# One kernel on Trainium2: expert weights in scaled fp16 halves, with the first matrix as the stationary operand

## The chip, the cores and the metric

The kernel runs on one core of a Trainium2 chip, as one program and one launch. The metric is the device time of an execution in microseconds (us); the result has to match the reference in float32.

## What is computed

Three parts follow one another: attention with 4 sink tokens and a window of 128, a dense MLP, and a mixture of 8 experts of which each token takes one. The change touches the third, with a piece of the second.

```python
# x: 3072 tokens x 512, out of attention (4 batches, 8 heads, 768 positions, head size 64)
h = x @ w_in; x = (h - np.tanh(h)) @ w_out           # 512 -> 2048 -> 512
logits = x @ w_gate + modality_bias[modality_id]     # 8 experts
e_idx = np.argmax(logits, axis=1); gate_w = ...      # softmax value of the chosen one
for e in range(E):
    mask = e_idx == e
    if not mask.any():
        continue
    h = np.maximum(x[mask] @ w1[e], 0.0)             # 512 -> 1024
    out[mask] = gate_w[mask, None] * (h @ w2[e])     # 1024 -> 512
```

With the inputs given, two of the eight experts get tokens, 1550 and 1522 of them.

## The kernel before

Attention and the dense MLP run in one block of 8 chunks (windows `w` = 0 to 7) of 384 tokens. A chunk has 32 slots `k`; in every second one an MLP step `f` begins: PE computes h_ps (L703), ACT takes tanh (L715), DVE the difference (L724), ACT and DVE its high and low fp16 halves (L734, L744), and PE adds g times w_out (L759). The routing of the chunk before, and attention of the next one, run beside it. SP's queue loads the eight raw pieces of the first expert's weights (`raw0` to `raw7`, 128x1024 float32, four of w1 and four of w2) in the last chunk.

Then comes the routing's end and a plan on DVE: `plan_blocks` and `plan_late` fill small tables (`meta`, `meta_late`) that tell for every block of 128 tokens which slots, which expert turn, and whether new weights are to be prepared. The block "experts" follows. Its engines take turns by semaphores; the order on each is that in which `iteration` calls the steps:

- `load_slots`, `gather` (POOL): slot numbers from DRAM, then an indirect DMA of 128 token rows into `xg`. `carry_waits` is a tiny POOL operation on `tick` that holds a wait before a DMA.
- `transpose_x`: 4 PE transposes into xt_ps (L1467), ACT copies the high part (L1472), DVE the remainder (L1475).
- `prep`: the weights of the next expert, split into a high and a low part in fp32r, ACT `w_hi` (L1429), DVE or POOL `w_lo` (L1432).
- `hidden` (L1498): 24 matmuls of 512 columns, tokens stationary, weights moving: low x high, high x low, high x high for each quarter of the depth and each half of the width.
- `hidden_transpose`: relu on ACT and DVE into `hid` (L1506, L1508), 8 transposes (L1519), and the halves `hid_hi` (L1527) and `hid_lo` (L1530).
- `output` (L1545): 24 matmuls of 512 columns, ACT scales by the gate value (L1551), POOL scatters the rows (L1556).

In an iteration `j` hidden of block `j` stands ahead of output of block `j - 1`. The weights lie in a buffer with two halves, chosen at run time: `par` is the parity of the expert turn, read from a table on each engine with `value_load` (helper `read`, L1405). A matmul on such a buffer takes its address from a register that instructions of the same engine compute. The loop is

```python
            with eng.Fori(2, NB) as j:       # L1605, NB = 31
                with eng.If(j <= last):      # L1606
                    block_step(E, eng, j)
```

`last` is 24 here (25 blocks), so that 6 passes of the loop are empty. In the tables of this document PE's queue of such instructions is PEldq, DVE's DVEq; FUSED_REGOPS and ALU_OP are register instructions, TENSOR_LOAD is the load of a table value.

Of the kernel before, what the change touches and what calls it, by code (L numbers as in the profile page):

```python
# [48 lines left out]
NB = NT + NE - 1  # L49
# [50 lines left out]
def attention_buffers(sb):  # L100
# [12 lines left out]
    words = 4 * QK + 2 * CT + 4 * KR + NB2 * DM + 2 * NB2 * HP * VW + 3 * DM + RING * KW + 6 * KW + 3 * P + 15 * P  # L113
    return (qk_raw, q_stack, kh_stack, kl_stack, v_raw, v_hi, v_lo, vs_raw, vs_hi, vs_lo, probs, normed, sinks, pt_hi, pt_lo), words


def front(nc, dram, shared, attention):

    with ExitStack() as ctx:
# [37 lines left out]
        ident = sb("ident", [P, P], F32)  # L157
# [743 lines left out]

        def gate_last(E, eng, g):
# [215 lines left out]
        def window(E, eng, w, first):  # L1118

            i = first  # L1120
            for k in range(SLOTS):
# [121 lines left out]
class Shared:  # L1243


    def __init__(self, sb, sem):
# [3 lines left out]
        self.early_int = sb("early_int", [1, 1], I32)  # L1250

# [10 lines left out]

    def over_attention(self, sb):

        self.raw = [sb(f"raw{i}", [P, FE], F32) for i in range(PIECES)]
        self.iota_t = sb("iota_t", [1, NT], F32)
# [8 lines left out]
        return PIECES * FE + NT + MB + NE + TURNS + 4 * MB + 5 * TURNS + TURNS * NT + 2 * MB * TURNS + 5 * MB  # L1275
# [15 lines left out]
    def plan(self, E, eng, counts):  # L1291
# [23 lines left out]
        step(ts(mv["active"][:], mv["blocks"][:], 0.0, None, ALU.is_gt))  # L1315
        step(eng.tensor_tensor_scan(mv["end"][:], self.one_x[:], mv["blocks"][:], 0.0, ALU.mult, ALU.add))
# [28 lines left out]
    def plan_late(self, eng):  # L1345
# [7 lines left out]
        first, now, b = vec["first"], metaf[:, 2, :], vec["b"]  # L1353
        step(ts(vec["t"][:], first[:], -1.0, 1.0, ALU.mult, ALU.add))
        step(ts(metaf[:, 2, :], first[:], 0.0, None, ALU.mult))
        step(tt(now[:, 1:MB], first[:, 0:MB - 1], first[:, 1:MB], ALU.mult))
        step(tt(b[:, 2:MB], first[:, 0:MB - 2], vec["t"][:, 1:MB - 1], ALU.mult))
        step(tt(now[:, 2:MB], now[:, 2:MB], b[:, 2:MB], ALU.add))
# [3 lines left out]
        step(tt(now[:, 1:MB], now[:, 1:MB], b[:, 0:MB - 1], ALU.mult))  # L1362
# [8 lines left out]
def experts(nc, dram, shared):  # L1371
# [5 lines left out]
    with ExitStack() as ctx:  # L1377
        sb, ps, sem = allocators(nc, ctx)
        tick, raw, q_raw = shared.tick, shared.raw, shared.raw_in
        w1_hi, w1_lo = (sb(n, [P, 2, KD, FE], F32R) for n in ("w1_hi", "w1_lo"))  # L1380
        w2_hi, w2_lo = (sb(n, [P, 2, KF, DM], F32R) for n in ("w2_hi", "w2_lo"))
# [3 lines left out]
        xg_hi, xg_lo = (sb(n, [P, DM], F32R) for n in ("xg_hi", "xg_lo"))  # L1385
        hid = sb("hid", [P, FE], F32)
        hid_hi, hid_lo = (sb(n, [P, FE], F32R) for n in ("hid_hi", "hid_lo"))
        y = sb("y", [P, DM], F32)
        ident = sb("ident2", [P, P], F32)
# [3 lines left out]
        ht_ps = [ps(f"ht_ps{i}", [P, 512], F32) for i in range(2)]  # L1393
        y_ps = ps("y_ps", [P, DM], F32)

        names = ("ident slot_in gathered xt_done xt_hi xt_lo "
                 "hid_mm relu_act relu_dve ht_done ht_hi ht_lo y_mm y_out scattered slot_y_in "
                 "ht_half carried_1 carried_2 carried_3").split()
        q = {n: sem("e_" + n) for n in names}
        q_hi, q_lo = ([sem(f"e_{x}{i}") for i in range(PIECES)] for x in ("hi", "lo"))  # L1400
# [5 lines left out]


        def load_turn(eng, s):
            e = read(eng, 3, s, NE - 1)
            for i in range(PIECES):  # L1410
                eng.wait_ge(q_lo[i], s)
                load_piece(eng, dram, shared, e, i)

        def piece(x_w1, x_w2, i, par):
            if i < KD:
                return x_w1[:, par, i, :] if isinstance(par, int) else x_w1[:, bass.ds(par, 1), i, :].rearrange("p a n -> p (a n)")
# [156 lines left out]
        def program(E, eng):  # L1573
# [13 lines left out]
            if E == "pe":  # L1587
                eng.wait_ge(q["ident"], 2)
# [108 lines left out]
```

## Time and profile before

| what | value |
|---|---|
| median of 3 runs | 1177.43 us (1176.83 to 1181.7) |
| profiled execution, its own time | 1180.4 us |
| its span | 1178.8 us |
| mean granted TensorE clock | 0.964 |
| PE busy | 1052.0 us, 89% of the span |
| PEld (weight loads) busy | 714.6 us, 61% |
| DVE busy | 690.8 us, 59% |
| ACT busy | 600.0 us, 51% |
| POOL busy | 414.6 us, 35% |

The span is that of one execution under the profiler, from the first to the last instruction. Busy times of an engine say how much it did, not whether anyone waited for it; that is told by the chain of waits, which follows the work that ended last back from the end. The whole-kernel table mixes stages: the experts take the last 350 us of it.

### The profile page before, as it was taken

The numbers are of one execution on the slowest core, as the hardware profiler recorded it, in microseconds if no ns is written. First come the engines' busy times: TensorE is split into PE (matmuls) and PEld (weight loads), VectorE is DVE, ScalarE is ACT, GpSimd is POOL, SyncE is SP. The second block draws the span as 40 slices with busy tenths as digits, with TensorE's granted clock in tenths as the row PEclk, the third lists the DMA queues.
The fourth block names the chain that finished last, engine by engine and source line by source line (L and its number), as shares of the span: only waits on it lengthen the run. The fifth ranks groups of instructions, "written<-read, shape, count | busy, mean of one in ns | idle before, by whom it ended". The sixth has DMA issues, their size and how long they took to land. (4 is left out here: it accounts for less than half of the span.)

```text
span 1178.8 us, 22058 instructions
## 1 busy us (share of the span) xinstructions
PE 1052.0 (89%) x6236; PEld 714.6 (61%) x6237; DVE 690.8 (59%) x2204; ACT 600.0 (51%) x1404; POOL 414.6 (35%) x469
## 2 busy tenths in 40 slices
PE   1667888999999999999999999995389999999996
PEld 0534554665665665665665666553277888888885
DVE  6787977678878778877777766334543222122221
ACT  2675866666686676676775765332332122122211
POOL 3796785123254223253322410002514222222221
PEclk9968999999999999999999999998689999999999
DMA  9731112312311421311321200400041111111111
GB/s 290 243 99 33 33 32 64 111 35 36 88 33 32 102 77 33 81 43 33 65 59 33 60 1 1 170 1 27 18 171 45 45 44 37 37 45 36 45 45 35
DMA packets 24245, 74.14 MB, mean 63 GB/s; under 512 B 10016, under 2 KB 10016, under 8 KB 22624
## 3 DMA queue, kind: packets, MB, share of 16 engines
q1 hardware_dynamic: 14768, 59.66, 18.9%
q0 software_dynamic: 5792, 13.43, 3.6%
q8 instruction: 40, 0.66, 0.3%
q10 hardware_dynamic: 3600, 0.03, 0.2%
q14 instruction: 45, 0.37, 0.1%
HBM read 60.04 MB, written 13.33 MB: 62 GB/s over the span
## 5 line engine op out<-in xcount | busy, mean ns | idle before, releaser
L759 PE MATMUL acc<-w_out_all,g_hi 128*128 128x512 f16 x768 | 228.3, 379 | 0.0
L703 PE MATMUL h_ps<-xt_hi,w_in_all 128*128 128x384 f16 x1024 | 211.0, 329 | 13.2 <-DVE g_raw L724 13.2
L759 PE MATMUL acc<-w_out_all,g_lo 128*128 128x512 f16 x384 | 145.4, 379 | 3.2 <-DVE g_lo L744 1.7
L703 PEld LDWEIGHTS h_ps<-xt_hi,w_in_all 128*128 128x128 f16 x1024 | 98.0, 98 | 73.1 <-issue 10.6
L591 ACT ACTIVATE pt_hi<-pt_ps 128x256 f16<-128x256 f32 (+2 forms) x224 | 83.5, 379 | 109.4 <-PE pt_ps L608 105.3
L97 POOL TENSOR_TENSOR tick<-tick 1x1 f32<-1x1 f32 x87 | 21.7, 249 | 317.1 <-ACT y L1551 114.4
L715 ACT ACTIVATE g_raw<-h_ps,batch_scale 128x384 f32<-128x384 f32 x128 | 74.2, 580 | 88.7 <-PE h_ps L703 87.4
L759 PEld LDWEIGHTS acc<-w_out_all,g_hi 128*128 128x128 f16 x768 | 75.0, 98 | 69.2
L744 DVE SCALAR_TENSOR_TENSOR g_lo<-g_raw,batch_scale,g_hi 128x384 f16<-128x384 f32 x128 | 95.1, 743 | 33.1 <-ACT g_hi L734 30.7
L595 DVE TENSOR_TENSOR pt_lo<-pt_ps,pt_hi 128x256 f16<-128x256 f32 (+2 forms) x224 | 94.3, 423 | 29.0 <-ACT pt_hi L591 27.2
L429 POOL TENSOR_TENSOR q_stack<-qk_raw,q_stack 64x768 f16<-64x768 f32 x31 | 50.8, 1637 | 165.6 <-ACT q_stack L425 165.6
L1530 DVE TENSOR_TENSOR hid_lo<-ht_ps,hid_hi 128x512 fp32r<-128x512 f32 x50 | 32.3, 686 | 127.6 <-ACT hid_hi L1527 127.6
L724 DVE SCALAR_TENSOR_TENSOR g_raw<-h_ps,batch_scale,g_raw 128x384 f32<-128x384 f32 x128 | 78.4, 613 | 48.7 <-ACT g_raw L715 47.7
L703 PE MATMUL h_ps<-xt_lo,w_in_all 128*128 128x384 f16 x512 | 106.1, 331 | 0.0
L572 ACT ACTIVATE normed<-probs,row_sum 128x260 f32<-128x260 f32 (+1 forms) x192 | 92.9, 484 | 20.5 <-DVE row_sum L567 20.4
L734 ACT ACTIVATE g_hi<-g_raw,batch_scale 128x384 f16<-128x384 f32 x128 | 78.0, 609 | 39.5 <-DVE g_raw L724 39.0
L554 ACT ACTIVATE probs<-probs,neg_max 128x260 f32<-128x260 f32 (+1 forms) x192 | 92.7, 483 | 5.8 <-DVE neg_max L549 5.7
L429 POOL TENSOR_TENSOR kl_stack<-qk_raw,kh_stack 128x1048 f16<-128x1048 f32 (+1 forms) x31 | 60.1, 1939 | 99.2 <-ACT kh_stack L425 98.9
L608 PE MATMUL pt_ps<-ident,normed 128*128 128x128 f32 x352 | 73.7, 285 | 22.3 <-ACT normed L572 22.3
L549 DVE CUSTOM_DVE_ANT_0 probs<-s_ps,mask 128x260 f32<-128x260 f32 (+1 forms) x180 | 73.1, 406 | 24.4 <-issue 23.2
L1545 PE MATMUL y_ps<-w_hi,hid_lo 128*128 x200 | 81.2, 406 | 2.6 <-DVE hid_lo L1530 2.6
L1551 ACT ACTIVATE y<-y_ps,slot_y 128x512 f32<-128x512 f32 x25 | 17.2, 687 | 124.5 <-PE y_ps L1545 124.5
(248 smaller groups left out, 2233.4 us busy)
## 6 DMA issues: line engine op xcount, KB each, us to landing
qk_raw<-in_qk SPq DMA_DIRECT2D x64, 454.0 KB, 6.0
raw<-in_w SPq DMA_DIRECT2D x16, 512.0 KB, 6.5
v_raw<-in_v SPq DMA_DIRECT2D x4, 1536.0 KB, 9.9
x_tokens<-x SPq DMA_DIRECT2D x24, 256.0 KB, 5.4
w_in_all<-in_w_in SPq DMA_DIRECT2D x4, 1024.0 KB, 13.2
w_out_all<-in_w_out SPq DMA_DIRECT2D x4, 1024.0 KB, 12.2
slot_g<-slots POOLq DMA_DIRECT2D x27, 1.0 KB, 2.0
xg<-x_tokens,slot_g POOLq DMA_INDIRECT x27, 3.4
```

What stands on the lines that cost most here:

```text
L429: eng.tensor_tensor(lo, raw[half], hi[half], ALU.subtract).then_inc(q["conv_lo"], 1)
L554: eng.activation(probs[:, r, cols], probs[:, r, cols], ACT.Exp, bias=neg_max[:, r:r + 1], scale=-1.0, accum_out=row_sum[:, r:r + 1]).then_ ...
L572: eng.activation(normed[:, u % 6, cols], probs[:, r, cols], ACT.Copy, scale=row_sum[:, r:r + 1])\
L591: eng.activation(pt_hi[:, at, :], out, ACT.Copy).then_inc(q["pt_hi_done"], 1)
L595: eng.tensor_tensor(pt_lo[:, at, :], out, pt_hi[:, at, :], ALU.subtract).then_inc(q["pt_lo_done"], 1)
L703: mm = eng.matmul(h_ps, w16[0][:, f, x * DM + k * P:x * DM + (k + 1) * P], r[:, par, k, :], start=(i == 0), stop=(i == 3 * KD - 1))
L715: eng.activation(g_raw[:, f % 2, :], h_ps, ACT.Tanh, scale=batch_scale[:, b, 0:1]).then_inc(q["tanh_done"], 1)
L724: eng.scalar_tensor_tensor(g, h_ps, batch_scale[:, b, 0:1], g, ALU.mult, ALU.subtract).then_inc(q["g_done"], 1)
L734: eng.activation(g_hi[f % 2][:], g, ACT.Copy, scale=batch_scale[:, b, 1:2]).then_inc(q["g_hi_done"], 1)
L744: eng.scalar_tensor_tensor(g_lo[f % 2][:], g, batch_scale[:, b, 1:2], g_hi[f % 2][:], ALU.mult, ALU.subtract)\
L759: mm = eng.matmul(acc[t][:, :], l[f % 2][:, t * P:(t + 1) * P], w16[1][:, f, x * DM:(x + 1) * DM], start=(f == 0 and i == 0), stop=(f == N ...
L1545: mm = eng.matmul(y_ps[:, :], l[:, f * P:(f + 1) * P], rhs, start=(f == 0 and i == 0), stop=(f == KF - 1 and i == 2))
```

## The change

Weights and activations of the experts are scaled by powers of two and kept as fp16 high and low halves. For this the kernel looks over each expert's weights (`look_over`: ACT sums squares of w1's pieces, DVE takes the largest magnitude of w2's), combines them across partitions (`sum_rows`, `spread` with two small matmuls) and makes scales (`set_scales`, eight small DVE operations). `split` makes the halves, ACT high and DVE low. Each gathered block gets a scale per token (`scale_x`), undone in the factor of the output (`output_scale`).

`hidden` now has w1 as the stationary operand and the tokens as the moving one, so its result is already transposed: 96 matmuls of 128 columns in place of 24 of 512; `hidden_transpose` is gone. `output` stands in the same iteration as its `hidden`. The first expert's weights are looked over and split in the last chunk of the MLP (`prepare_expert`, slots 9 to 21); the second expert's in `look_ahead`, `scale_ahead` and `split_ahead` over three iterations, each behind a table read and a branch. `plan_late` runs before the first iteration, and all engines wait for it. An expert with tokens gets at least two blocks, and `NB` becomes 38.

```diff
-NB = NT + NE - 1
+NB = NT + 2 * NE - 2
...
+        def prepare_expert(E, eng, k):
+
+            if k in (9, 11):
+                for i in (k - 9, k - 8):
+                    shared.look_over(E, eng, 0, i)
+            if k == 11:
+                shared.sum_rows(E, eng, 0)
+            if k == 13:
+                shared.spread(E, eng, 0, pt_bank[0])
+                shared.set_scales(E, eng, 0, pt_bank[0])
+            if k in (15, 17, 19, 21):
+                shared.split(E, eng, 0, (k - 15, k - 14))
...
+                if w == NC - 1:
+                    prepare_expert(E, eng, k)
...
+    def look_over(self, E, eng, s, i):
+
+        if E == "act":
+            eng.wait_ge(self.raw_in[i], 16 * (s + 1))
+            need(eng, self.rows_set, 2 * s)
+            eng.activation(self.junk[:, i, :], self.raw[i][:], ACT.Square, accum_out=self.sums[:, i:i + 1])\
+               .then_inc(self.squared, 1)
+        if E == "dve":
+            eng.wait_ge(self.raw_in[KD + i], 16 * (s + 1))
+            eng.tensor_reduce(self.tops[:, i:i + 1], self.raw[KD + i][:], AX.X, ALU.max,
+                              apply_absolute_value=True).then_inc(self.maxed, 1)
...
+    def spread(self, E, eng, s, bank):
+
+        if E == "pe":
+            eng.wait_ge(self.rows_set, 2 * (s + 1))
+            need(eng, self.scaled, s)
+            for i in range(2):
+                mm = eng.matmul(bank[:, P * i:P * (i + 1)], self.rows[:, i:i + 1].to_broadcast([P, P]), self.ident[:],
+                                start=True, stop=True)
+            mm.then_inc(self.spread_done, 1)
+
+    def set_scales(self, E, eng, s, bank):
+
+        if E != "dve":
+            return
+        eng.wait_ge(self.spread_done, s + 1)
...
+        step(eng.tensor_reduce(self.both[:], bank[:, 0:2 * P].rearrange("p (i n) -> p i n", i=2), AX.X, ALU.max))
+        step(ts(exps[:], self.both[:].bitcast(I32), 255 * EXP1, None, ALU.bitwise_and))
+        step(ts(exps[:, 0:1], exps[:, 0:1], float(147 * EXP1), 0.5, ALU.add, ALU.mult))
...
+        step(ts(self.w_scale[:].bitcast(I32), exps[:], -1.0, float((254 + TOP16) * EXP1), ALU.mult, ALU.add))
...
+    def split(self, E, eng, s, pieces):
+
+        for i in pieces:
+            scale = self.w_scale[:, 0:1] if i < KD else self.w_scale[:, 1:2]
+            hi, lo = (self.piece(x, i, s % 2) for x in (self.hi, self.lo))
+            if E == "act":
+                eng.wait_ge(self.scaled, s + 1)
+                eng.activation(hi, self.raw[i][:], ACT.Copy, scale=scale).then_inc(self.w_hi[i], 1)
+            if E == "dve":
+                eng.wait_ge(self.scaled, s + 1)
+                eng.wait_ge(self.w_hi[i], s + 1)
+                eng.scalar_tensor_tensor(lo, self.raw[i][:], scale, hi, ALU.mult, ALU.subtract).then_inc(self.w_lo[i], 1)
...
+        def scale_x(E, eng, j):
+
+            if E == "dve":
+                step = chain(eng, q["x_step"], 4 * j)
+                ts = eng.tensor_scalar
+                eng.wait_ge(q["gathered"], 16 * (j + 1))
+                need(eng, q["x_scaled"], j)
+                if not (isinstance(j, int) and j < 2):
+                    eng.wait_ge(q["y_set"], j - 1)
+                step(eng.tensor_reduce(x_top[:], xg[:], AX.X, ALU.max, apply_absolute_value=True))
+                step(ts(x_exp[:], x_top[:].bitcast(I32), 255 * EXP1, None, ALU.bitwise_and))
+                step(ts(x_exp[:], x_exp[:], float(2 * EXP1), float(253 * EXP1), ALU.max, ALU.min))
+                step(ts(x_scale[:].bitcast(I32), x_exp[:], -1.0, float(255 * EXP1), ALU.mult, ALU.add))
+                ts(column(x_undo, j % 2).bitcast(I32), x_exp[:], float(-EXP1), None, ALU.add).then_inc(q["x_set"], 1)
+            if E == "act":
+                eng.wait_ge(q["x_set"], j + 1)
+                eng.activation(xg[:], xg[:], ACT.Copy, scale=x_scale[:]).then_inc(q["x_scaled"], 1)
...
+        def hidden(E, eng, j, s):
+
+            for c in range(2):
+                if E == "pe":
+                    par = s % 2
+                    if c == 0:
+                        eng.wait_ge(q["xt_lo"], j + 1)
+                    if not (isinstance(j, int) and j == 0):
+                        eng.wait_ge(q["hid_lo"], 2 * j - 1 + c)
+                    for f in range(4 * c, 4 * c + 4):
+                        i = 0
+                        for x, w in ((xg_lo, shared.hi), (xg_hi, shared.lo), (xg_hi, shared.hi)):
+                            for k in range(KD):
+                                if c == 0 and f == 0 and i < KD:
+                                    eng.wait_ge(shared.w_lo[k], s + 1)
+                                mm = eng.matmul(hid_ps[c][:, (f - 4 * c) * P:(f - 4 * c + 1) * P],
+                                                shared.piece(w, k, par)[:, f * P:(f + 1) * P], x[:, k * P:(k + 1) * P],
+                                                start=(i == 0), stop=(i == 3 * KD - 1))
+                                i += 1
+                    mm.then_inc(q["hid_mm"], 1)
+                half = slice(c * 512, (c + 1) * 512)
+                if E == "act":
+                    eng.wait_ge(q["hid_mm"], 2 * j + c + 1)
+                    need(eng, q["y_mm"], j)
+                    eng.activation(hid_hi[:, half], hid_ps[c][:, :], ACT.Relu).then_inc(q["hid_hi"], 1)
+                if E == "dve":
+                    eng.wait_ge(q["hid_hi"], 2 * j + c + 1)
+                    eng.scalar_tensor_tensor(hid_lo[:, half], hid_ps[c][:, :], 0.0, hid_hi[:, half], ALU.max, ALU.subtract)\
+                       .then_inc(q["hid_lo"], 1)
...
-                    for i, (l, r) in enumerate(((hid_lo, w2_hi), (hid_hi, w2_lo), (hid_hi, w2_hi))):
-                        rhs = r[:, par, f, :] if isinstance(par, int) else r[:, bass.ds(par, 1), f, :].rearrange("p a n -> p (a n)")
+                        eng.wait_ge(shared.w_lo[KD + f // 2], s + 1)
+                    for i, (l, w) in enumerate(((hid_lo, shared.hi), (hid_hi, shared.lo), (hid_hi, shared.hi))):
+                        rhs = shared.piece(w, KD + f // 2, par)[:, (f % 2) * DM:(f % 2 + 1) * DM]
...
-        def iteration(E, eng, j, turn, turn_before):
-
-            load_slots(E, eng, j + 2)
-            prep_ahead(E, eng, j, range(KD))
-            hidden(E, eng, j, turn)
-            transpose_x(E, eng, j + 1)
-            prep_ahead(E, eng, j, range(KD, PIECES))
-            gather(E, eng, j + 2)
-            if turn_before is not None:
-                load_slots_again(E, eng, j - 1)
-                output(E, eng, j - 1, turn_before)
-            hidden_transpose(E, eng, j)
+        def iteration(E, eng, j, ago_1, ago_2):
+
+            turn = 0 if isinstance(j, int) and j == 0 else read(eng, 1, j, NE) if E in ("pe", "dve") else None
+            if E == "pe":
+                hidden(E, eng, j, turn)
+                scale_ahead(E, eng, ago_1)
+                transpose_x(E, eng, j + 1)
+                output(E, eng, j, turn)
+            if E == "act":
+                hidden(E, eng, j, turn)
+                transpose_x(E, eng, j + 1)
+                load_slots_again(E, eng, j)
+                split_ahead(E, eng, j, ago_2, range(KD, PIECES))
+                look_ahead(E, eng, j)
+                split_ahead(E, eng, j, ago_1, range(2))
+                output(E, eng, j, turn)
+                scale_x(E, eng, j + 2)
+                split_ahead(E, eng, j, ago_1, range(2, KD))
+            if E == "dve":
+                hidden(E, eng, j, turn)
+                transpose_x(E, eng, j + 1)
+                output_scale(E, eng, j, turn)
+                split_ahead(E, eng, j, ago_2, range(KD, PIECES))
+                look_ahead(E, eng, j)
+                scale_ahead(E, eng, ago_1)
+                scale_x(E, eng, j + 2)
+                split_ahead(E, eng, j, ago_1, range(KD))
...
+            if E == "dve":
+                shared.plan_late(eng)
...
             transpose_x(E, eng, 0)
             eng.wait_ge(shared.planned, 1)
             last = read(eng, 1, MB - 1, NB - 1, lo=NT - 1)
             load_slots(E, eng, 1)
             gather(E, eng, 1)
-            prep(E, eng, 0, 0, range(KD, PIECES))
-            if E == "dve":
-                shared.plan_late(eng)
-            iteration(E, eng, 0, 0, None)
-            if E in ("act", "dve", "pool"):
-                eng.wait_ge(shared.planned_late, 1)
-            block_step(E, eng, 1)
+            scale_x(E, eng, 1)
+            eng.wait_ge(shared.planned_late, 1)
+            iteration(E, eng, 0, None, None)
+            iteration(E, eng, 1, 0, None)
             with eng.Fori(2, NB) as j:
                 with eng.If(j <= last):
-                    block_step(E, eng, j)
-            load_slots_again(E, eng, last)
-            output(E, eng, last, read(eng, 1, last, NE) if E == "pe" else 0)
+                    iteration(E, eng, j, j - 1, j - 2)
             if E == "pool":
```

PE, in the loop body, within `hidden`: one k-step of before (ISA and REGISTER_ALU are register instructions; `ew_hi`, `ew_lo` are the halves of the weights).

```order
L1498 ISA
L1498 MATMUL hid_ps<-w_hi,xg_lo 128x512
L1498 ISA
L1498 MATMUL hid_ps<-w_hi,xg_lo 128x512
L1498 REGISTER_ALU
L1498 MATMUL hid_ps<-w_lo,xg_hi 128x512
L1498 REGISTER_ALU
L1498 MATMUL hid_ps<-w_lo,xg_hi 128x512
L1498 MATMUL hid_ps<-w_hi,xg_hi 128x512 x2
L1464 ISA
L1467 MATMUL xt_ps<-ident,xg 128x128 x4
```

And of the change, one of its eight groups `f`.

```order
L1602 ISA
L1602 MATMUL hid_ps<-xg_lo,ew_hi 128x128
L1602 REGISTER_ALU
L1602 MATMUL hid_ps<-xg_hi,ew_lo 128x128
L1602 REGISTER_ALU
L1602 MATMUL hid_ps<-xg_hi,ew_lo 128x128
L1602 REGISTER_ALU
L1602 MATMUL hid_ps<-xg_hi,ew_lo 128x128
L1602 REGISTER_ALU
L1602 MATMUL hid_ps<-xg_hi,ew_lo 128x128
L1602 MATMUL hid_ps<-xg_hi,ew_hi 128x128 x4
L1602 ISA
```

A step of before has 2 ISA and 2 REGISTER_ALU for 6 matmuls of 512 columns, four steps in all; the change has 4 ISA and 4 REGISTER_ALU for 12 matmuls of 128 columns, eight groups in all.

DVE, in the loop body of the change, behind xg_lo: `output_scale`, and the first of the reads of `meta_late` with its branch.

```order
L1627 ISA
L1629 ISA
L1629 TENSOR_TENSOR y_scale<-slot_y,x_undo 128x1
L1632 ISA
L1632 TENSOR_TENSOR y_scale<-y_scale,ew_undo 128x1
L1499 ISA
L1499 TENSOR_LOAD meta_late
L1499 ISA x2
L1529 COMPARE_AND_BRANCH
```

And `scale_x` in the same body.

```order
L1558 ISA
L1562 TENSOR_REDUCE x_top<-xg 128x1
L90 ISA
L1563 TENSOR_SCALAR x_exp<-x_top 128x1
L90 REGISTER_ALU
L1564 TENSOR_SCALAR x_exp<-x_exp 128x1
L90 REGISTER_ALU
L1565 TENSOR_SCALAR x_scale<-x_exp 128x1
L90 REGISTER_ALU
L1566 ISA
L1566 TENSOR_SCALAR x_undo<-x_exp 128x1
```

Neither stood on DVE before, which had two table reads in an iteration there, and now has five.

## Rows read from the trace of the kernel before

**Rows 1.** Chain of waits over the experts: start us, us, what.

```profile
837.57 3.41 DMA xg<-x_tokens,slot_g
...
846.00 6.02 DVE w_lo L1432 x2
...
858.82 8.55 PE hid_ps L1498 x24
867.80 5.61 PE y_ps L1545 x24
...
906.38 5.61 PE y_ps L1545 x24
...
924.51 0.88 PE ht_ps L1519 x8
925.39 5.61 PE hid_ps L1498 x24
930.99 0.44 PE xt_ps L1467 x4
```

**Rows 2.** Busy time by stretch: a steady period, and part of the last chunk.

```profile
core 0: us, PE busy (x) PEld busy (x) DVE busy (x) ACT busy (x) POOL busy (x), PEclk, DMA share, GB/s
950.42:962.95 12.53, 12.53 (x61) 10.23 (x61) 2.67 (x4) 2.76 (x6) 3.15 (x6) 1.00 0.14 42
...
780.00:808.00 28.00, 27.18 (x149) 14.24 (x147) 11.22 (x35) 7.70 (x15) 3.10 (x4) 1.00 0.01 1
```

**Rows 3.** PE's queue, line 1498: duration ns min/median/max, first and last start us.

```profile
L1498 PEldq FUSED_REGOPS  x8: 46/46/94, 962.2 to 963.9; - x8
L1498 PEldq ALU_OP  x8: 32/32/32, 962.5 to 964.1; - x8
```

**Rows 4.** PE's queue, line 1545, the last output; columns as in rows 3.

```profile
L1545 PEldq ALU_OP  x8: 32/32/32, 1165.9 to 1167.8; - x8
```

**Rows 5.** Timeline of PE: start us, us, engine line op out<-in xcount.

```profile
52.06 1.08 PE L279 MATMUL acc<-w_out_all 128*128 128x128 bf16 x16
52.98 0.22 PE L539 MATMUL s_ps<-kl_stack,q_stack 128*128 128x132 f16 x1
```

**Rows 6.** Timeline of a step of the last chunk, PE and ACT.

```profile
748.58 0.38 PE L759 MATMUL acc<-w_out_all,g_lo 128*128 128x512 f16 x1
...
748.78 0.58 ACT L715 ACTIVATE g_raw<-h_ps,batch_scale 128x384 f32<-128x384 f32 x1 [1.94 <-PE h_ps L703]
...
749.23 0.38 PE L759 MATMUL acc<-w_out_all,g_lo 128*128 128x512 f16 x1
...
752.67 0.58 ACT L715 ACTIVATE g_raw<-h_ps,batch_scale 128x384 f32<-128x384 f32 x1 [2.01 <-PE h_ps L703]
```

**Rows 7.** PE's queue, lines 1605 and 1405, one turn; columns as in rows 3.

```profile
L1605 PEldq ALU_OP  x1: 32/32/32, 972.3 to 972.3; - x1
...
L1405 PEldq TENSOR_LOAD <-meta x2: 298/299/300, 973.0 to 973.8; - x2
```

**Rows 8.** Groups by form on DVE: xcount, busy us, mean ns, idle before.

```profile
L1530 DVE TENSOR_TENSOR hid_lo<-ht_ps,hid_hi 128x512 fp32r<-128x512 f32 x50 | 32.3, 686 | 127.6 <-ACT hid_hi L1527 127.6
...
L452 DVE TENSOR_REDUCE v_top<-v_raw 128x1 f32<-128x512 f32 x24 | 16.3, 678 | 1.0 <-DMA v_raw<-in_v 0.8
...
L397 DVE TENSOR_SCALAR qk_scale<-qk_scale 128x1 int32<-128x1 int32 x32 | 4.9, 153 | 1.1
...
L432 DVE SCALAR_TENSOR_TENSOR kl_stack<-qk_raw,qk_scale,kh_stack 128x792 f16<-128x792 f32 x1 | 1.0, 1030 | 0.0
```

**Rows 9.** DVE's queue, line 1405, one read; columns as in rows 3.

```profile
L1405 DVEq TENSOR_LOAD <-meta_late x1: 312/312/312, 964.5 to 964.5; - x1
```

**Rows 10.** Timeline of POOL before the first gather.

```profile
833.46 3.95 POOL L97 TENSOR_TENSOR tick<-tick 1x1 f32<-1x1 f32 x1 [0.79 <-DMA slot_g<-slots]
```

**Rows 11.** Timeline of PE, the last matmul.

```profile
1171.37 0.39 PE L1545 MATMUL y_ps<-w_hi,hid_hi 128*128 x1
```

**Rows 12.** DVE's queue, line 1605, empty passes of the loop; columns as in rows 3.

```profile
L1605 DVEq ALU_OP  x6: 40/40/40, 1164.9 to 1168.5; - x6
```

More of the change, by code:

```diff
@@ L1261, in __init__ @@
         self.blocks_step = sem("plan_blocks_step")
+        self.squared = sem("squared")
+        self.maxed = sem("maxed")
+        self.rows_set = sem("rows_set")
+        self.spread_done = sem("spread_done")
+        self.scale_step = sem("scale_step")
+        self.scaled = sem("scaled")
+        self.w_hi = [sem(f"ew_hi{i}") for i in range(PIECES)]
+        self.w_lo = [sem(f"ew_lo{i}") for i in range(PIECES)]
     def over_attention(self, sb):
         self.raw = [sb(f"raw{i}", [P, FE], F32) for i in range(PIECES)]
+        self.hi, self.lo = (sb(n, [P, 2, PIECES, FE], F16) for n in ("ew_hi", "ew_lo"))
+        self.junk = sb("junk", [P, KD, FE], BF16)
+        self.sums = sb("sums", [P, KD], F32)
+        self.tops = sb("tops", [P, PIECES - KD], F32)
+        self.rows = sb("rows", [P, 2], F32)
+        self.both = sb("both", [P, 2], F32)
+        self.exps = sb("exps", [P, 2], I32)
+        self.w_scale = sb("ew_scale", [P, 2], F32)
+        self.undo = sb("ew_undo", [P, TURNS], F32)
         self.iota_t = sb("iota_t", [1, NT], F32)
@@ L1350, in plan_late @@
         turns = mv["turn_end"][:, TURNS - 1:TURNS]
[L1353 to L1358, printed above, removed]
+        b = vec["b"]
         step(ts(b[:], metaf[:, 1, :], 1.0, None, ALU.add))
@@ L1361, in plan_late @@
         step(tt(b[:], b[:], vec["t"][:], ALU.mult))
-        step(tt(now[:, 1:MB], now[:, 1:MB], b[:, 0:MB - 1], ALU.mult))
+        step(tt(metaf[:, 2, :], vec["first"][:], b[:], ALU.mult))
         step(tt(grid["a"][:], mv["turn_end"][:].unsqueeze(1).to_broadcast([1, MB, TURNS]), self.iota_j[:].unsqueeze(2).to_broadcast([1, MB, TURNS]), ALU.is_le))
@@ L1378, in experts @@
         sb, ps, sem = allocators(nc, ctx)
-        tick, raw, q_raw = shared.tick, shared.raw, shared.raw_in
-        w1_hi, w1_lo = (sb(n, [P, 2, KD, FE], F32R) for n in ("w1_hi", "w1_lo"))
-        w2_hi, w2_lo = (sb(n, [P, 2, KF, DM], F32R) for n in ("w2_hi", "w2_lo"))
+        tick, ident = shared.tick, shared.ident
         slot_g = sb("slot_g", [P, 2], I32)
@@ L1510, in hidden_transpose, with output_scale @@
[L1510 to L1531 removed]
+        def output_scale(E, eng, j, s):
+            if E == "dve":
+                eng.wait_ge(q["slot_y_in"], 16 * (j + 1))
+                need(eng, q["y_out"], j)
+                eng.tensor_tensor(y_scale[:], slot_y[:, 1:2].bitcast(F32), column(x_undo, j % 2), ALU.mult)\
+                   .then_inc(q["y_step"], 1)
+                eng.wait_ge(q["y_step"], j + 1)
+                eng.tensor_tensor(y_scale[:], y_scale[:], column(shared.undo, s), ALU.mult).then_inc(q["y_set"], 1)
@@ L1549, in output @@
                 eng.wait_ge(q["y_mm"], j + 1)
-                eng.wait_ge(q["slot_y_in"], 16 * (j + 1))
-                eng.activation(y[:], y_ps[:, :], ACT.Copy, scale=slot_y[:, 1:2].bitcast(F32)).then_inc(q["y_out"], 1)
+                eng.wait_ge(q["y_set"], j + 1)
+                eng.activation(y[:], y_ps[:, :], ACT.Copy, scale=y_scale[:]).then_inc(q["y_out"], 1)
             if E == "pool":
@@ L1591, in program @@
             gather(E, eng, 0)
-            prep(E, eng, 0, 0, range(KD))
+            if E == "dve":
+                shared.plan_late(eng)
+            scale_x(E, eng, 0)
             transpose_x(E, eng, 0)
```

166 lines of the change are left out of this document (63 added, 103 removed).

## The prediction

> **What bounds the kernel now.** I read the page, then the chain of waits over the experts, then single queues. The chain shows a part to 829.8 us that the change hardly touches, a start in which conversions are in the way, and a steady state where one TensorE group follows another: hid_ps 5.61, y_ps 5.61, ht_ps 0.88, xt_ps 0.44 us, so 12.52 us per block of 128 tokens [rows 1]. In one such period PE is busy throughout, at a granted clock of 1.00, with DVE at 2.67 us, ACT at 2.76 and POOL at 3.15 [rows 2]. The array bounds the blocks; whatever takes columns off it pays until another limit is reached. The next one can be seen: the sequencer that feeds PE. For the 24 hidden matmuls it carries out 16 register instructions (8 FUSED_REGOPS, 8 ALU_OP), from 962.2 to 964.1, some 2.02 us with the last matmuls [rows 3]. The last output, where nothing holds it, takes it 2.4 us for as many (the ALU_OPs start from 1165.9 to 1167.8 [rows 4]). Now it does this ahead of an array that needs 5.61 us.
>
> **The array after the change.** Hidden: 96 matmuls of 128 columns for 24 of 512, the same 12,288 columns, each with a weight load of its own. Static 128-column bf16 matmuls with their own loads run 16 from 52.06 to 52.98, 57 ns apart [rows 5]: 96 x 0.057 = 5.5 us for 5.61. Output: an fp16 matmul of 512 columns takes 0.216 us, three from 748.58 to 749.23 [rows 6], for 0.234: 24 x 0.216 = 5.2, a gain of 0.4. The ht_ps transposes go, 0.88. The array needs 5.5 + 5.2 + 0.44 = 11.1 us per block for 12.52.
> The Trainium skill, page "TensorE: Matmul & The Clock Gate", section "Back-to-back issue gap", gives about 81 ns per matmul for a stream of load and matmul pairs at 128 columns. Row 5 says 57; the page's figure is weighed among the rivals.
>
> **The sequencer after the change.** In the new order each group of 12 hidden matmuls carries 4 ISA and 4 REGISTER_ALU, so 64 for 96 matmuls where there were 16 for 24: everything is fourfold. So I need not split the cost between register instructions and matmuls: 4 x 2.02 = 8.1 us [rows 3], and 4 x 2.4 = 9.6 if the output's pace holds [rows 4]. The rest of its period: loop turn 0.6 (from 972.3 to the next read, whose load starts at 973.0 [rows 7]), a table read, 0.8, since two TENSOR_LOADs start 0.8 apart [rows 7], with 0.3 of address work behind it; in the middle the new read and branch of scale_ahead, which PE does nowhere yet, taken at a read and 0.2 for the branch, 1.0; waits and xt_ps 0.2; output 2.4. Sum 0.6 + 0.8 + 0.3 + 8.1 + 1.0 + 0.2 + 2.4 = 13.4 us. The array's backlog cannot help: it has its 11.1 us done while the sequencer takes 13.4. **Period 13.4 us.** From below 12.6, with 4 x 1.9 for hidden (first to last start [rows 3]) and 0.8 for the read and branch, 0.1 off the rest; from above 15.0, by 9.6 and the waits.
>
> **Other engines in the period.** DVE: two hid_lo and xg_lo 3 x 0.69 [rows 8], five reads with their branches 4.6 (its TENSOR_LOAD takes 312 ns [rows 9], PE's 299 in a read of 0.8; with a branch I take 0.92), scale_x 0.68 for the 512-wide reduce [rows 8] and four small operations at 0.2 (153 ns and a gap [rows 8]), y_scale 0.4, loop 0.7: 9.3 us, under 13.4. ACT has as many reads and five operations of DVE's length or less, and is no longer. The new chain of gather (3.41 us to land [rows 1]), scale_x 1.5, multiply 0.6 starts at xt_ps of one block and has until the next: 6 us of slack. Output can no longer lie a block behind hidden; what covers its hid_lo (ACT 0.6, DVE 0.69, 1.5 us with waits) is the read, xt_ps and the first half of output, 2.4 us of sequencer time. Cost nothing, up to 0.3 if that cover is thin.
>
> **The last chunk.** DVE gets two looks or two splits over 128x1024 (1.2 and 1.3 us, estimates by the reduce of 512 columns at 0.68 and the two-operand form of 792 at 1.03 [rows 8]) in slots 9, 11, 15, 17, 19 and 21. One MLP step of two slots is 3.89 us (tanh to tanh [rows 6]), and from 780 to 808 DVE is busy 11.22 of 28 [rows 2], 2.3 us free per step; but it lies in two gaps of under 2 us, before g_raw and before g_lo, for which PE waits. 2.4 to 2.6 us of work overfills it by 0.3 to 0.6 us, five or six times: **+2.5 us**, between 0.5 and 5. ACT's squares and copies at 1.0 are less. The raw loads are there before slot 9.
>
> **The start of the experts.** Now the first gather waits for a tick of 3.95 us beside DVE's w_lo [rows 10], then 3.41 for the landing; DVE has w_lo until 852.0, then plan_late; y_ps(0) ends at 873.4 [rows 1]. After: no tick held (-3.7), scale_x +2.1, xt and converts 2.4: hidden(0) from about 842.3, with static addresses; it and output(0) take 5.5 + 5.2 us and about 1 for a clock that has fallen (hid_ps(1) took 8.55 for 5.61 [rows 1]): y(0) ends near 854.1. Plan_late now runs during the gather, shorter by five operations, but every engine waits for it.
> Then the second expert's weights: SP can load only after plan_late, DVE gets 4 looks, sums and scales, and 8 splits: 4 x 1.2 + 2.1 + 8 x 1.3 = 17.3 us over blocks 1 to 3. With 9.3 of its own per block that is 3 x 9.3 + 17.3 = 45.2, part of it under block 0; I take 44.2 for these three, where 3 x 13.4 = 40.2: y(3) ends at 898.3, with the last chunk's 2.5 at **900.8**. Before it ends at 912.0 [rows 1], after a stall for POOL's w_lo and a late gather. Gain 11.2 us, between 7 and 15.
>
> **The 21 blocks from there.** Before: 912.0 to the last y_ps's end at 1171.8 [rows 1, 11], 259.8 us (20 periods and a last output by itself). After: 21 x 13.4 = 281.4. **+21.6**; 264.6 to 315 by the bounds, +5 to +55.
>
> **The tail.** Before: 7.0 us from the last matmul to the end at 1178.8 [rows 11], through ACT's y and POOL's scatter. NB is now 38, so 13 empty passes for 6. On DVE an empty pass is 0.71 us (from 1164.9 to 1168.5 for six starts [rows 12]), formerly under the last output. Now output is inside the loop: DVE has four reads and scale_x after hid_lo, done about 3 us behind the last matmul, then 13 x 0.71 = 9.2, then 1 to leave: 13.4. **+6.4**, between 3 and 8. PE's 13 x 0.73 from its sequencer's lead gives less.
>
> **Sum.** -11.2 + 21.6 + 6.4 = +16.8 us (2.5 of the last chunk is in the first term). On the profiled execution, span 1178.8 and 1180.4 in all, that is 1195.6 of span. The median of the runs shown is 1177.43, 3 us below it; the difference carries over: 1177.4 + 16.8 = **1194 us**.
>
> **Rivals.**
> *The array stays the bound (faster).* The sequencer's 2.02 us were measured while it could run, but it may be paced there by a full queue of matmuls rather than by register work. For: alone, a FUSED_REGOPS is 46 ns and an ALU_OP 32 [rows 3], and 64 of them at 40 ns are 2.6 us, less than the array's 5.5. Against: the 16 starts in 1.9 us are an even 0.12 apart, in a sequencer that is then ahead of the array, and the last output, where its queue was empty, is no faster [rows 3, 4]. It decides below 0.09 us per register instruction (8.1 would be 5.8, the array's pace). Then the period is 11.1 to 12.0 (hid_lo's latency shows): 21 x 11.6 = 244, -16, with stalls of blocks 1 to 3 unchanged -11.2, tail +6.4: 1156, 1150 to 1166. Chance 0.14.
> *A cheaper sequencer.* Period 12.5 to 12.95, around the low bound: 1175 to 1185 (each 0.1 us of it is 2.1). Chance 0.14.
> *Pairs are paced by the weight load.* If each fp16 pair with other operands than row 5's took half as long again, hidden would be 96 x 0.08 = 7.7 us and the array 13.3: 1192, hardly another time by another mechanism, told by even spacing of the matmuls with no gaps at register instructions. Chance 0.07, in the forecast's range. The page named above gives this: 96 x 81 ns = 7.8 us.
> *Dearer issue.* Pace of row 4 in hidden, or code fetched anew each turn, since a PE turn has twice the instructions: period 14 to 15, 1207 to 1228. Chance 0.13. Or the granted clock falls from 1.00 with the gaps.
> *The two-block rule for an expert* changes nothing here: the inputs give 1550 and 1522 tokens to two experts, 13 and 12 blocks, so no padding block comes. The change does what it says.
>
> **How the numbers follow.** Forecast (period 13.0 to 13.9) 0.52, with the load-paced rival 0.59; cheaper 0.14; dearer 0.13; array-bound 0.14. The range leaves out the array-bound case and the top of the dearer one: 1168 to 1212. 0.5% is about what a measurement of this kernel can tell from none. Faster by over 0.5% (below 1171.5): 0.14; slower (above 1183.3): the forecast, load-paced, dearer, and 0.02 of the cheaper: 0.74; within: 0.12.
>
> **What would show it.** Right: in a steady period hid_ps matmuls in bursts with gaps, their group 7.5 to 8.5 us long, PE's register instructions of the hidden line 64 per block at 0.12 us, PE idle put down to issue, y_ps 5.2 us, y_ps starts 13.4 apart; ACT and DVE waiting for PE; y(3) ending near 901; 13 DVE passes closing the span. Wrong: hid_ps in 5.5 us; a period under 12.5; DVE named as releaser of hid_ps in the steady state; chunk 7 longer than 3 us more or unchanged; a stall at blocks 1 to 3 over 10 us.

## The result: 1195.8 us, and the profile after

The changed kernel takes 1195.81 us in the median of 4 runs (1191.55 to 1199.68), the kernel before 1177.26 (1176.83 to 1181.7). The ratio is 1.0148, with a 95% interval of 1.0105 to 1.0191: slower by 1.5%. The forecast was 1194 us, 1168 to 1212, with a chance of 0.74 for slower. The profiled execution took 1196.78 us with a span of 1195.0, for which the prediction had 1195.6.

| | before | after | forecast |
|---|---|---|---|
| experts begin | 829.8 | 832.1 | +2.5 |
| y_ps(0) ends | 873.4 | 863.3 | 856.6 |
| y_ps(3) ends | 912.0 | 904.9 | 900.8 |
| period of a block | 12.52 | 13.21 | 13.4 |
| last y_ps ends | 1171.8 | 1182.4 | 1182.2 |
| from there to the end | 7.0 | 12.6 | 13.4 |

On the profile's page of the changed kernel PE is busy for as long as before, to 0.3%, in a span that is 16 us longer.

```profile
span 1195.0 us, 27235 instructions
...
PE 1048.7 (88%) x7844; PEld 684.4 (57%) x7845; DVE 731.0 (61%) x2392; ACT 620.8 (52%) x1422; POOL 401.1 (34%) x463
```

The chain of waits in the steady state (start us, us, what). It answers to [rows 1]: ht_ps is gone and y_ps is shorter, but hid_ps takes 6.58 us for 5.61, and 0.81 us of issue stand behind it.

```profile
984.19 6.58 PE hid_ps L1602 x96
990.77 0.81 issue
991.58 0.63 PE xt_ps L1577 x4
992.21 5.18 PE y_ps L1646 x24
```

The same period by windows (PE, PEld, DVE, ACT, POOL busy, PEclk, DMA share, GB/s). PE now has gaps, at a clock of 1.00; no other engine is busy for more than 3.7 us (register instructions and branches are not counted as busy), for 3.15 us before [rows 2].

```profile
core 0: us, PE busy (x) PEld busy (x) DVE busy (x) ACT busy (x) POOL busy (x), PEclk, DMA share, GB/s
992.21:1005.44 13.23, 12.39 (x125) 8.99 (x124) 3.70 (x10) 3.20 (x5) 3.15 (x6) 1.00 0.13 40
```

One `hidden` in PE's timeline. A row is four matmuls; the rows of `xg_lo,ew_hi` open one of the eight groups of 12 each. From 985.37 to 986.04 and 986.71 a group takes 0.67 us, 55.8 ns a matmul. From then on the groups stand 0.94, 0.98 and 0.99 us apart: what the sequencer had put in the queue is used up, and the array goes at the sequencer's pace. Within such a group the matmuls with register instructions ahead of them take 0.38 and 0.39 us for four (988.63 to 989.01 to 989.40). The last four, which have none of their own, take 0.22, the pace of the array.

```profile
985.37 0.39 PE L1602 MATMUL hid_ps<-xg_lo,ew_hi 128*128 128x128 f16 x4
...
986.04 0.39 PE L1602 MATMUL hid_ps<-xg_lo,ew_hi 128*128 128x128 f16 x4
...
986.71 0.41 PE L1602 MATMUL hid_ps<-xg_lo,ew_hi 128*128 128x128 f16 x4
...
987.65 0.45 PE L1602 MATMUL hid_ps<-xg_lo,ew_hi 128*128 128x128 f16 x4
...
988.63 0.45 PE L1602 MATMUL hid_ps<-xg_lo,ew_hi 128*128 128x128 f16 x4
989.01 0.55 PE L1602 MATMUL hid_ps<-xg_hi,ew_lo 128*128 128x128 f16 x4
989.40 0.38 PE L1602 MATMUL hid_ps<-xg_hi,ew_hi 128*128 128x128 f16 x4
989.62 0.45 PE L1602 MATMUL hid_ps<-xg_lo,ew_hi 128*128 128x128 f16 x4
```

PE's queue in that stretch (duration ns min/median/max, first and last start us), which answers to [rows 3]: 22 register instructions start within 2.6 us, 0.12 us for each on average, with their matmuls in between.

```profile
L1602 PEldq ALU_OP  x12: 32/32/32, 987.9 to 990.2; - x12
...
L1602 PEldq FUSED_REGOPS  x10: 46/46/46, 987.6 to 989.7; - x10
```

The start, in the chain of waits. Block 1's gather takes 6.99 us to land, for the 3.72 of block 0's and the 3.41 of [rows 1], and y_ps(0) runs 7.04 us for 5.18. The granted clock was 0.51 from 845 to 850 and 0.50 from 857 to 860, in the first parts of hid_ps(0) and y_ps(0), and 1.00 in the steady state.

```profile
845.68 6.99 DMA xg<-x_tokens,slot_g
852.70 0.70 DVE x_top L1562
...
856.23 7.04 PE y_ps L1646 x24
863.27 6.65 PE hid_ps L1602 x96
...
899.73 5.18 PE y_ps L1646 x24
```

The end: the last matmul, and DVE's loop instruction in its 13 empty passes and the exit, 0.69 us apart. It answers to [rows 11, 12].

```profile
1181.98 0.38 PE L1646 MATMUL y_ps<-ew_hi,hid_hi 128*128 x1
```

```profile
L1717 DVEq ALU_OP  x14: 40/40/40, 1185.6 to 1194.6; - x14
```

### The profile page after: what moved, and what is told of

Read it like the earlier page. It is cut to its first block and busy times, and to the rows that moved or that the text cites. A ratio compares the mean times of both kernels' runs of the same rounds, so it can differ in the third digit from the quotient of the medians.

```text
span 1195.0 us, 27235 instructions
## 1 busy us (share of the span) xinstructions
PE 1048.7 (88%) x7844; PEld 684.4 (57%) x7845; DVE 731.0 (61%) x2392; ACT 620.8 (52%) x1422; POOL 401.1 (34%) x463
## 5 line engine op out<-in xcount | busy, mean ns | idle before, releaser
L97 POOL TENSOR_TENSOR tick<-tick 1x1 f32<-1x1 f32 x87 | 17.2, 198 | 349.9 <-DVE payload L878 113.5
L1602 PE MATMUL hid_ps<-xg_hi,ew_lo 128*128 128x128 f16 x800 | 95.8, 219 | 0.0
L1614 DVE SCALAR_TENSOR_TENSOR hid_lo<-hid_ps,hid_hi 128x512 f16<-128x512 f32 x50 | 34.3, 691 | 91.8 <-ACT hid_hi L1611 91.8
L1602 PE MATMUL hid_ps<-xg_lo,ew_hi 128*128 128x128 f16 x800 | 85.1, 222 | 1.5 <-DVE xg_lo L1585 1.5
```

Of the source, the lines that this page charges most:

```text
L1602: mm = eng.matmul(hid_ps[c][:, (f - 4 * c) * P:(f - 4 * c + 1) * P], shared.piece(w, k, par)[:, f * P:(f + 1) * P], x[:, k * P:(k + 1) * P ...
```

## Experiments

"Fixed" below is an address known when the program is built. Times of single executions stand beside 1180.53 us for the kernel before on the same chip (1180.33 in the second set, 1178.95 in the third). Single executions of the changed kernel lie up to 8 us apart (1191.55 to 1199.68), so that a few us in the time of one say little; periods, which repeat over some 20 blocks within 0.1 us, say more.

**All of hidden at fixed addresses**

```diff
-                    par = s % 2
+                    par = 0
```

> The changed kernel, but hidden always takes its weights from the first half of the buffer, at addresses known when the program is built (so the second expert's tokens are multiplied by the first expert's w1). Its 64 register instructions per block go; output keeps its 16. My theory, that PE's sequencer sets the period of 13.2 us: it has some 8 us per block left or less, the array 11.1, so y_ps starts come 11.1 to 11.8 us apart and the time falls by 30 to 48 us, to about 1155. Rival, that pairs of weight load and 128-column matmul are slow in themselves: period 13.0 to 13.3, no change in time.

1155.22 us; y_ps starts are 11.25 to 11.29 us apart. Its chain of waits:

```profile
994.33 5.36 PE hid_ps L1602 x96
999.69 0.13 issue
999.82 0.63 PE xt_ps L1577 x4
1000.45 5.18 PE y_ps L1646 x24
```

Only the addresses have changed, and with them the 64 register instructions per block are gone: hid_ps takes 5.36 us, 96 matmuls at 55.8 ns, with 0.13 of issue behind them. The matmuls themselves are not slow. The rival of slow pairs falls. So does any by which another engine sets the period: ACT, DVE and POOL do the same work as in the changed kernel, in 11.27 us.

**Two of eight groups at fixed addresses**

```diff
-                                                shared.piece(w, k, par)[:, f * P:(f + 1) * P], x[:, k * P:(k + 1) * P],
+                                                shared.piece(w, k, 0 if f in (3, 7) else par)[:, f * P:(f + 1) * P], x[:, k * P:(k + 1) * P],
```

> As the last, but only two of hidden's eight groups have fixed addresses: 48 register instructions for 64. Sequencer theory: a fixed group costs 0.3 to 0.7 us of it for 0.98 now, so the period falls by 0.6 to 1.3 us, to 11.9 to 12.6, and the time by 13 to 29 us. Rival of slow pairs: no change.

1158.85 us, period 11.49 to 11.60, below the 11.9 to 12.6 that I expected. In the chain of waits hid_ps and the issue behind it are still over the level of the array:

```profile
994.33 5.50 PE hid_ps L1602 x96
999.83 0.19 issue
1000.02 0.63 PE xt_ps L1577 x4
1000.64 5.18 PE y_ps L1646 x24
```

As some issue time is left, the sequencer still bounds this kernel or nearly so. Sixteen register instructions less save 13.21 - 11.55 = 1.66 us, at least 0.104 us each. A fixed group of 12 then costs the sequencer at most 0.98 - 0.83 = 0.15 us, 0.83 being eight register instructions at 0.104. The matmuls that I carried along in "everything is fourfold" are a small part of it. "Register instruction" stands here for the instruction together with the matmul that takes its address; what each of the two costs alone isn't shown.

**Four of eight groups at fixed addresses**

```diff
-                                                shared.piece(w, k, par)[:, f * P:(f + 1) * P], x[:, k * P:(k + 1) * P],
+                                                shared.piece(w, k, 0 if f % 2 else par)[:, f * P:(f + 1) * P], x[:, k * P:(k + 1) * P],
```

> Four of the eight groups with fixed addresses, 32 register instructions. Sequencer theory: twice the step of the run with two groups, until the array's 11.1 us end it: period 11.1 to 12.0. Rival of slow pairs: no change. A fall that is not in proportion before the array's level would speak for a queue effect and against a fixed price per register instruction.

1156.47 us, period 11.25 to 11.31 (in these three runs the fixed groups take the first expert's w1 for both experts, so that its part for the second expert is left out). The second 16 instructions bring 0.25 us, since the array's level is reached: 5.36 + 5.18 + 0.63 and a gap of 0.1. Period against register instructions of hidden is 13.21 (64), 11.55 (48), 11.30 (32), 11.27 (0): a fall and then a floor, as with two resources of which the slower one counts. Only two of the points lie above the floor, so that a fixed price per register instruction isn't shown.

**Hidden written twice, behind a branch on the parity (everything computed)**

`hidden_of` is PE's part of `hidden` with the half of the buffer as a constant.

```diff
...
+                    with eng.If(s % 2 < 1):
+                        hidden_of(eng, j, s, 0)
+                    with eng.If(s % 2 > 0):
+                        hidden_of(eng, j, s, 1)
```

> The changed kernel with hidden written twice, for each half of the buffer with fixed addresses, and a branch on the parity that takes one of them; everything is computed. Sequencer theory: like the run with the fixed half, plus some 0.3 us for two branches that the backlog covers: period 11.1 to 11.9, time 1150 to 1168, ratio to the kernel before 0.975 to 0.99. Rival of slow pairs: ratio as for the change, 1.015. If longer code makes instruction fetch late, the gain shrinks and PE idles behind the branch by over 0.5 us per block.

1156.88 us (4 runs), ratio to the kernel before 0.9795 (0.977 to 0.9819): faster than both kernels. The period is 11.53 to 11.58 us in blocks of the first expert and 11.25 to 11.30 in those of the second. For the first expert the second body is jumped over behind hidden, where the queue is running empty:

```profile
996.25 5.36 PE hid_ps L1600 x96
1001.61 0.34 issue
1001.95 0.65 PE xt_ps L1577 x4
```

0.34 us of issue here, and 0.08 for the second expert, for which the jump lies ahead of hidden, where the backlog of y_ps covers it.

**The loop's end read at run time**

```diff
-            with eng.Fori(2, NB) as j:
-                with eng.If(j <= last):
-                    iteration(E, eng, j, j - 1, j - 2)
+            with eng.Fori(2, last + 1) as j:
+                iteration(E, eng, j, j - 1, j - 2)
```

> The changed kernel with the loop's end at last + 1, read at run time, in place of NB = 38 with a test in every pass: no empty passes. If the 13 empty passes on DVE make the tail, the time from the last matmul to the end falls from 12.6 us to 4 to 5, and the time by 8 to 11 us in all, with up to 0.2 us less per pass. If the scatter and its drain make the tail: 7 us or more stay.

1192.12 us, 1190.4 of span: 4.6 us less, for the 8 to 11 that I expected. Period 13.13 to 13.18, 0.05 less. From the last matmul to the end it is 7.0 us, as in the kernel before and not the 4 to 5 of my expectation. So the empty passes cost 5.6 us, and behind them stood, unseen, the scatter with its drain. Tail and periods make 6.7 us; 2.2 of them went at the start, where y_ps(3) began at 901.95 for 899.73 in this one execution.

**The kernel before with 13 empty passes**

```diff
-NB = NT + NE - 1
+NB = NT + 2 * NE - 2
```

> The kernel before with NB = 38: 13 empty passes instead of 6. There they run under the last output, so that seven more at 0.7 us end at about 1173.5 on DVE, ahead of the drain at 1176: 0 to +0.5 us behind the last matmul. The rival, that an empty pass costs its 0.7 us anywhere: +5 us.

1186.78 us, a span of 1185.2 for 1178.8: +6.4 us where I expected 0 to 0.5. I had looked at DVE. PE's timeline shows that the last output, which stands behind the loop, has to wait for PE's own empty passes, the last at 1169.2, with a table read behind them. It begins 14.31 us behind the output before it, for 9.10 in the kernel before:

```profile
1161.58 1.04 PE L1519 MATMUL ht_ps<-ident,hid 128*128 128x128 f32 x8
1170.45 0.79 PE L1545 MATMUL y_ps<-w_hi,hid_lo 128*128 x1 [7.83 <-issue]
1171.04 0.63 PE L1545 MATMUL y_ps<-w_lo,hid_hi 128*128 x1
```

PE is idle for 7.83 us, and its first matmuls after that are 0.43 us apart instead of 0.234, at a granted clock of 0.50 (1170.5 to 1174.4).

**Block 1's scale behind block 0's hidden**

```diff
-            scale_x(E, eng, 1)
             eng.wait_ge(shared.planned_late, 1)
...
                 hidden(E, eng, j, turn)
+                if isinstance(j, int) and j == 0:
+                    scale_x(E, eng, 1)
                 transpose_x(E, eng, j + 1)
```

> The changed kernel with the scale of block 1's tokens taken after block 0's hid_hi and hid_lo instead of before, so that block 0 does not wait for the 6.99 us landing of block 1's gather. y_ps(0) starts 2.5 to 4 us earlier, at 852 to 853.7 for 856.23. If DVE's work for the second expert sets blocks 1 to 3, under 2 us of it are left at the end of y_ps(3) (904.9 now); if not, all of it.

1199.19 us. In this run all started 1.8 us later; from the first matmul of hid_ps(0) to that of y_ps(0) it took 11.4 to 11.6 us, as before (844.65 to 856.23 there). I had expected it 2.5 to 4 us sooner. The chain of waits names who is late:

```profile
854.59 0.69 DVE x_top L1562
...
856.05 0.73 ACT xg L1569
...
856.83 1.12 PE xt_ps L1577 x4
857.95 6.08 PE y_ps L1646 x24
```

On PE the transposes of block 1 stand ahead of output(0), so that the late gather holds output in any order of DVE and ACT.

**The first expert prepared at the start of the experts**

```diff
-                if w == NC - 1:
-                    prepare_expert(E, eng, k)
...
+            for i in range(KD):
+                shared.look_over(E, eng, 0, i)
+            shared.sum_rows(E, eng, 0)
+            shared.spread(E, eng, 0, stat_ps)
+            shared.set_scales(E, eng, 0, stat_ps)
+            shared.split(E, eng, 0, range(PIECES))
```

> The changed kernel without the first expert's preparation in the last chunk: looks, scales and splits come at the start of the experts, before the first tokens are scaled. The experts begin 2.0 to 2.5 us earlier (832.1 now, about 829.8 then); DVE has 17 us of weight work ahead of scale_x(0), so hidden(0) starts at 856 to 860 for 844.7: the time rises by 8 to 13 us. If the chunk's DVE work had been free, the first part would show no difference.

1208.18 us, 11.3 more in the span. The experts begin at 829.6, hid_ps(0) at 859.53. As expected: in these two executions this part of the change costs 2.5 us where it stands and saves 14.9 at the start of hidden.

**All of PE's block written twice, with the loop's end at run time**

`side` is hidden, scale_ahead, the transposes and output on PE, with the half of the buffer as a constant.

```diff
...
+                with eng.If(turn % 2 < 1):
+                    side(eng, j, turn, 0, ago_1)
+                with eng.If(turn % 2 > 0):
+                    side(eng, j, turn, 1, ago_1)
...
+            with eng.Fori(2, last + 1) as j:
```

> The changed kernel with all of PE's work of a block written twice, once for each half of the weight buffer with fixed addresses, behind a branch on the parity, and the loop's end at last + 1 instead of empty passes. Sequencer theory: the array alone sets the period, 11.2 to 11.35 us for both experts (11.54 and 11.26 with hidden alone written twice, where the skipped body's branch fell into the gap before xt_ps); against that run 12 x 0.27 = 3 us less, and 5.6 us less at the tail, as the run with the loop's end showed: 1146 to 1150, ratio to the kernel before 0.970 to 0.977. If the branch costs as much elsewhere, the first expert's period stays at 11.5.

1144.9 us (5 runs, 1142.8 to 1146.08), ratio to the kernel before 0.9714 (0.9692 to 0.9736), about 1 us below what I expected. The period is 11.25 to 11.31 for both experts, the gap before xt_ps 0.12:

```profile
987.52 5.36 PE hid_ps L1600 x96
992.88 0.12 issue
993.00 0.63 PE xt_ps L1577 x4
993.63 5.18 PE y_ps L1649 x24
```

This is the best version: 51 us below the changed kernel, 34 below the one before. The jump over the other body, now behind y_ps, does not show in the period of either expert.

**The same, with the second expert's loads behind block 1's gather**

```diff
                 eng.wait_ge(shared.planned_late, 1)
+                eng.wait_ge(q["gathered"], 32)
```

> As two_sides, but SP loads the second expert's weights only when block 1's tokens have landed. The landing of block 1's gather then takes 3.4 to 4 us for 6.99, and y_ps(0) starts 2.5 to 3.5 us earlier after hid_ps(0) starts (8.1 to 9 us for 11.6). Whether it is kept: if DVE's work for the second expert sets blocks 1 to 3, y_ps(3) ends no earlier, and the later loads may cost up to 2 us; else 2 to 3 us less in all.

1149.2 us (4 runs), ratio to the kernel before 0.9746 (0.972 to 0.9772): 4 us worse than the version before it. The landing is short, 4.2 us from its issue at 843.6, and y_ps(0) starts at 852.57, 8.3 us behind hid_ps(0), as expected. But the loads now begin at 849.5. The small slot_y transfer beside them takes 7.21 us, DVE, which needs it for y_scale, comes to its four looks and to block 2's scale later, and y_ps(1) starts only at 870.0, for 864.9 in the version before:

```profile
853.49 7.21 DMA slot_y<-slots
...
870.01 7.02 PE y_ps L1649 x24
```

What block 0 gained, blocks 1 to 3 paid back and more; here it is right to load early.

**The kernel before with the loop's end at run time**

```diff
-            with eng.Fori(2, NB) as j:
-                with eng.If(j <= last):
-                    block_step(E, eng, j)
+            with eng.Fori(2, last + 1) as j:
+                block_step(E, eng, j)
```

> The kernel before with the loop's end at last + 1 in place of NB = 31 with a test in every pass. Its last output stands behind the loop on PE, so that the empty passes held it (with 13 of them PE sat idle 7.83 us ahead of it, and its first matmuls ran at half the clock): now y_ps(24) starts 1 to 2 us sooner, ratio 0.998 to 1.0. If the six passes cost nothing today, no difference. Either way it stays 20 us or more above the changed kernel with fixed addresses.

1178.03 us (10 runs), ratio 0.9983 (0.9964 to 1.0002): no difference that can be told from none. y_ps(24) starts 7.91 us behind y_ps(23), for 9.10 (1156.79 to 1165.89) in the kernel before, 1.2 us sooner:

```profile
1164.29 0.50 PE L1545 MATMUL y_ps<-w_hi,hid_lo 128*128 x1 [1.44 <-DVE hid_lo L1530]
```

So the loop's end is worth about 1 us to the kernel before by its trace, within what the times can tell, and the best version stays 33 us below it. In the changed layout the same edit takes away the 5.6 us that the empty passes had added there.

## Why the prediction was right, step by step

**The sequencer bounds the period: right, and shown.** The forecast was 13.4 us, measured 13.21. The runs with 48, 32 and no register instructions in hidden tell it from slow pairs: on the same matmuls the period goes to 11.27. One sign that I had named did not come: hid_ps was to be 7.5 to 8.5 us long, and it is 6.58, with 0.81 of issue behind it. The sequencer begins hidden while the array still works off y_ps, so that the first four of its eight groups run at the array's pace. The array's 11.1 us were 5.36 + 5.18 + 0.63 = 11.17. "Everything is fourfold" gave 8.1 us for hidden; eight groups at 0.98 are 7.8. The 0.2 us of error are that, with the rest of the sequencer's turn at 5.4 for 5.3. Scaling by four held for a reason that I had not separated: register instructions at 0.10 us or more carry nearly all of it, fixed matmuls almost nothing. It would have failed for a change that multiplies one and not the other.

**The rival by which the array stays the bound** named the right level (11.1 to 12.0) for the state without that work. Its argument was wrong: 46 and 32 ns are what the records show, and the price in the stream is 0.10 to 0.12 us.

**Slow pairs.** They take 55.8 ns per load and matmul of 128 columns in fp16, near the 57 that [rows 5] had for bf16. The Trainium skill, page "TensorE: Matmul & The Clock Gate", section "Back-to-back issue gap", has about 81 ns for such a stream; the runs disagree, and the measurement decides.

**The last chunk: right by luck for the start of the experts, too low for the chunk.** The experts begin 2.3 us later, for 2.5. But from the tanh at 741.04 to that at 803.16 it is 62.1 us before, and from 739.66 to 805.88 it is 66.2 after, so 4.1 us for my 2.5. By the prediction's own list, "chunk 7 longer than 3 us more" was a sign of being wrong. The looks and splits were sized right on DVE (1.21 and 1.28 us each, for 1.2 and 1.3); what they push out of a step was taken too low. The changed kernel's chunk had begun 1.4 us earlier in its run, and this hid most of it. The chunk is 62.1 us in all four profiles without this part and 66.2 in all nine with it, while its beginning moves by up to 4 us among the nine; why stays open. Single steps took up to 5.8 us for 3.9, as here with 5.1:

```profile
768.54 0.58 ACT L714 ACTIVATE g_raw<-h_ps,batch_scale 128x384 f32<-128x384 f32 x1 [0.18 <-PE h_ps L702]
...
773.68 0.58 ACT L714 ACTIVATE g_raw<-h_ps,batch_scale 128x384 f32<-128x384 f32 x1 [3.00 <-PE h_ps L702]
```

The run without that part, whose chunk takes 62.1 us and whose experts begin at 829.6, shows that it is the cause. That it is DVE's share and not ACT's is argued from the gaps, not shown.

**The start: one term missing, one too low.** hid_ps(0) began at 844.65, where the forecast with the chunk's 2.5 gives 844.8 (842.3; its terms as written add up to 841.8). y_ps(0) ended 6.7 us later than forecast. I had not priced block 1's gather beside the second expert's loads, which plan_late now releases earlier (6.99 us; some 3 us of wait; 4.2 us in the run that holds these loads back, which shows that they are the cause). The half clock I had priced at 1 us in all; it came in both hid_ps(0) and y_ps(0), 8.0 and 7.04 us for 5.5 and 5.2. Blocks 1 to 3 won part of it back: they took 41.6 us for 44.2. DVE's four looks and eight splits for the second expert took 4.6 and 9.8 us, for 4.8 and 10.4. Net y_ps(3) was 4.1 us later, and the gain 7.1 us for 11.2, at the low bound.

**The tail: right by its number, incomplete in its causes.** +5.6 for +6.4. The empty passes of DVE set it (its terms, 3 + 9.2 + 1, add up to 13.2 us and not to the 13.4 written there; measured 12.6). In the kernel before I took the empty passes for hidden under the last output. They were not: PE's own passes delayed the start of that output against the run without any, by 1.2 us with six and by 6.4 with 13. The six are part of the measured time before, and so the forecast did not suffer.

**The sum.** -7.1 + 17.7 + 5.6 = +16.2 us of span, for -11.2 + 21.6 + 6.4 = +16.8. The terms were off by +4.1, -3.9 and -0.8 us, and the first two cancelled: that the number came this close is luck, and it is better than the working. The direction is not luck: the largest term, 17.7 us, is 21 times the longer period, and the runs show what makes it longer.

## What to carry to other kernels

Count the instructions that an engine's sequencer must carry out beside those for the array, and price the turn as a whole from a stretch in which the queue was free. Matmuls on a smaller tile with run-time addresses multiply them, here from 16 to 64 in hidden. Where the run-time value has two cases, two bodies with fixed addresses behind a branch on it take that work away, and the jump belongs where the array still has a backlog. Empty passes of a loop count on every engine that has work behind the loop, not only on the last to leave.

## What the runs showed of the hardware that was not expected

- Register instructions on PE, each with the matmul that takes its address, cost the stream 0.10 to 0.12 us though their records show 32 to 46 ns; a pair of load and matmul at fixed addresses costs the sequencer at most 0.0125 us (0.15 us for 12), worked out from the periods 13.21 and 11.55.
- An idle stretch of 7.83 us on PE was followed by matmuls of 512 columns 0.43 us apart for ten of them, at a granted clock of 0.50, then 0.23 at 1.00: the wait cost another 2 us.
- A gather of 128 rows took 6.99 us beside eight loads of 512 KB, 3.4 to 4.2 without them; a transfer of 1 KB took 7.21 beside them, 1.7 at the last block of the changed kernel.
- A branch that jumps over 96 matmuls cost 0.27 us per block where the array waited for it (11.54 for 11.27), and nothing that shows where it had a backlog. Whether the branch itself or the fetching of what follows takes the time isn't shown.
